# Payload rows as floats with both gates, multiplied and split per block on GpSimd, ScalarE and VectorE

## What is computed

```python
# x: (4, 3584, 192) -> attention -> (14336, 192)
logits = x @ phi                                 # 32 slots
d = softmax(logits, axis=0); c = softmax(logits, axis=1)
slot_out = experts(d.T @ x)                      # 8 experts, 4 slots each
x = c @ slot_out
noisy = x @ w_gate + log1p(exp(x @ w_noise)) * noise
top2, top2_w = two largest of noisy, softmax of the two
out[row] = sum over k of top2_w[row, k] * (relu(x[row] @ w1[e]) @ w2[e])
```

## Time and profile before

| | busy us | share of the span |
|---|---|---|
| TensorE matmul | 1046.8 | 91% |
| VectorE | 634.6 | 55% |
| ScalarE | 440.8 | 38% |
| GpSimd | 324.4 | 28% |

### The profile page before, as it was taken

One profiled execution on the slowest core, in us unless ns is written; L12 is line 12 of the kernel. 1 busy time (PEld: TensorE's weight loads), 2 busy tenths in 40 slices (PEclk: granted clock), 3 DMA queues, 4 the chain that ended last, 5 costly groups with the idle time before them and its releaser, 6 DMA issues.

```text
span 1149.5 us, 27573 instructions
## 1 busy us (share of the span) xinstructions
PE 1046.8 (91%) x8758; PEld 812.1 (71%) x8759; DVE 634.6 (55%) x1091; ACT 440.8 (38%) x818; POOL 324.4 (28%) x347
## 2 busy tenths in 40 slices
PE   6999899887886087999999999999999999999996
PEld 6999899713632035777777777777777777777774
DVE  3232542450379994656656655665666556655663
ACT  2222212110022453445544554454445444544453
POOL 4000000100001903443344334343433343334431
PEclk9999999989777588999999999999999999999999
DMA  6456765646242222333333333333333333333331
GB/s 203 154 177 205 248 198 200 192 132 194 59 110 62 120 99 59 112 109 109 109 106 112 109 106 106 108 113 104 109 111 103 113 106 112 110 106 106 111 113 39
DMA packets 76143, 142.29 MB, mean 124 GB/s; under 512 B 10876, under 2 KB 37804, under 8 KB 73800
## 3 DMA queue, kind: packets, MB, share of 16 engines
q1 hardware_dynamic: 64072, 120.72, 34.8%
q0 software_dynamic: 11120, 20.51, 6.1%
q10 hardware_dynamic: 912, 0.52, 0.2%
HBM read 67.70 MB, written 19.37 MB: 76 GB/s over the span
## 4 chain that ended last, share of the span: by engine, by line
PE 85%; DVE 6%; DMA 5%; issue 1%; ACT 1%; another core or an unknown queue 0%; POOL 0%; SPq 0%; PEldq 0%; ACTq 0%; POOLq 0%; DVEq 0%
PE ps L1156 32%; PE ps L1160 16%; PE ps L1145 11%; PE ps L950 8%; DMA stage<-in_moe_w 5%; PE ps L999 3%; PE ps L943 3%; PE ps L1001 2%; PE ps L1120 2%; PE ps L1031 2%; PE ps L1099 2%; PE ps L1135 1%; PE ps L1047 1%; PE ps L1082 1%; DVE gbuf L811 1%
## 5 line engine op out<-in xcount | busy, mean ns | idle before, releaser
L901 DVE SCALAR_TENSOR_TENSOR x_ring<-ps,x_ring 128x512 f16<-128x512 f32 x556 | 356.4, 682 | 275.4 <-ACT x_ring L557 163.6
L557 ACT ACTIVATE x_ring<-ps 128x512 f16<-128x512 f32 x556 | 302.4, 599 | 366.2 <-PE ps L1145 279.1
L1156 PE MATMUL ps<-w2hl,x_ring 128*128 x2224 | 408.7, 326 | 2.7 <-issue 1.4
L1156 PEld LDWEIGHTS ps<-w2hl,x_ring 128*128 128x128 f16 x2224 | 207.7, 97 | 113.8 <-issue 6.4
L444 POOL DMA_INDIRECT out_rows<-x_ring,row_id x139 | 137.2, 987 | 387.7 <-DVE x_ring L910 382.7
L1160 PE MATMUL ps<-w2hl,x_ring 128*128 x2224 | 228.9, 246 | 0.0
L1160 PEld LDWEIGHTS ps<-w2hl,x_ring 128*128 128x128 f16 x2224 | 191.3, 98 | 36.4 <-DVE x_ring L901 1.8
L1145 PE MATMUL ps<-c,x_ring 96*128 96x128 f16 x2224 | 170.9, 219 | 0.0
L438 POOL DMA_INDIRECT stage<-pay_rows,row_id x139 | 134.8, 970 | 77.5 <-DVE row_id L888 35.4
L1145 PEld LDWEIGHTS ps<-c,x_ring 96*128 96x128 f16 x2224 | 140.9, 98 | 0.0
L950 PE MATMUL ps<-phi_r,xT 96*128 96x224 f32 (+6 forms) x616 | 106.1, 321 | 0.0
(11 more groups left out here) (209 smaller groups left out, 651.1 us busy)
## 6 DMA issues: line engine op xcount, KB each, us to landing
x_ring<-a SPq DMA_DIRECT2D x278, 192.0 KB
stage<-in_moe_w SPq DMA_DIRECT2D x48, 768.0 KB, 7.9
x_ring<-in_x SPq DMA_DIRECT2D x14, 1536.0 KB, 6.6
pay_rows<-x_ring SPq DMA_DIRECT2D x4, 1344.0 KB, 4.6
stage<-pay_rows,row_id POOLq DMA_INDIRECT x139, 2.5
out_rows<-x_ring,row_id POOLq DMA_INDIRECT x139
gbuf<-in_moe_noise ACTq DMA_DIRECT2D x1, 448.0 KB, 5.7
x_halo<-in_x SPq DMA_DIRECT2D x4, 72.0 KB, 3.6
```

The source lines that it names most:

```text
L557: a.activation(hh[:, par, 4 * half:4 * half + 4, :].rearrange("p j q -> p (j q)"), ps[:, 2 + 2 * par + half, :], ACT.Relu).then_inc(hh_rea ...
L901: last = v.scalar_tensor_tensor(hl[:, par, 4 * half:4 * half + 4, :].rearrange("p j q -> p (j q)"), ps[:, 2 + 2 * par + half, :], 0.0, hh[ ...
L1156: t_.matmul(ps[:, 6 + b % 2, 0:2 * D], hh[:, k, j, :], w, start=k == 0 and j == 0, stop=False)
```

## The change

The payload row becomes 34 floats (136 bytes): the 32 numbers of c and the two gates. ScalarE copies lg into the tile cg (that takes the place of the payload quarters) and GpSimd writes the gates beside it from a reciprocal that VectorE leaves after the block tables; one DMA stores all. GpSimd also takes over the remainder of a3 from VectorE, reading a float copy a_f that ScalarE makes. The transposes of lg (quads) move between the steps of the earlier weights, into tiles of their own.

In the last loop GpSimd multiplies the gathered 32 numbers by both gates (gated, 128x64), ScalarE rounds and writes the result twice (split_high), VectorE subtracts (split_low); each stands LEAD = 3 blocks ahead of the block it serves. turn_c waits for split_low instead of the gather. In the changed kernel relu is L566, low_sum L572, split_high L579, low L893, row_sum L902, c_out L886, split_low L908, gather L441, multiplication L451, scatter L457.

```diff
         stage2 = sb("stage2", [P, T * NS])
         w2s = stage2[:, 0:2 * FJ * D].rearrange("p (a j d) -> p a j d", a=2, d=D)
-        ck = stage2[:, :].rearrange("p (a k t s) -> p a k t s", a=2, k=2, s=NS)
-        crow = stage2[:, 0:CR * KS].bitcast(F16).rearrange("p (a k) -> p a k", a=CR)
+        crow = stage2[:, 0:CR * KP].rearrange("p (a k) -> p a k", a=CR)
+        ck = stage2[:, CR * KP + 4 * KS:CR * KP + 4 * KS + 8 * NS].rearrange("p (a k s) -> p a k s", a=4, k=2)
+        csp = stage2[:, CR * KP:CR * KP + 4 * KS].bitcast(F16).rearrange("p (a k r s) -> p a k r s", a=4, k=2, s=NS)
         ident = sb("ident", [P, P])
...
-            sp.dma_start(pay[N:ROWS, :].rearrange("(p a) k -> p (a k)", a=4), zero16[:, :]).then_inc(zero_rows, 16)
-            for q in range(QT):
-                sp.wait_ge(pay_lo, 2 * q + 2)
-                sp.dma_start(pay[0:N, :].rearrange("(p t) k -> p t k", t=T)[:, q * TQ:(q + 1) * TQ, :],
-                             payload[:, q % 2, :, :]).then_inc(pay_out[q % 2], 16)
+            sp.dma_start(pay[N:ROWS, :].rearrange("(p a) k -> p (a k)", a=4),
+                         zero16[:, 0:2 * 4 * KP].bitcast(F32)).then_inc(zero_rows, 16)
+            sp.wait_ge(cg_ready, 1)
+            sp.wait_ge(gates_ready, 2)
+            sp.dma_start(pay[0:N, :].rearrange("(p t) k -> p t k", t=T), cg[:, :, :]).then_inc(pay_out, 16)
...
-            for a in range(2):
-                sp.wait_ge(pay_out[a], 8 * QT)
+            sp.wait_ge(pay_out, 16)
...
-            pool.wait_ge(gates_ready, 1)
-            def gated(q):
-                if q >= 2:
-                    pool.wait_ge(pay_lo, 2 * q - 2)
-                ts = slice(q * TQ, (q + 1) * TQ)
-                for k in range(2):
-                    g.tensor_tensor(ck[:, q % 2, k, :, :], lg[:, PAD + q * TQ:PAD + (q + 1) * TQ, :],
-                                    gm[:, 4 + k, ts].unsqueeze(2).to_broadcast([P, TQ, NS]), ALU.mult
-                                    ).then_inc(ck_ready, 1)
-            gated(0)
-            for q in range(QT):
-                if q + 1 < QT:
-                    gated(q + 1)
-                pool.wait_ge(ck_ready, 2 * q + 2)
-                for k in range(2):
-                    pool.wait_ge(pay_hi, 2 * q + k + 1)
-                    row = payload[:, q % 2, :, k * KS:(k + 1) * KS]
-                    g.tensor_tensor(row[:, :, 2 * NS:3 * NS], ck[:, q % 2, k, :, :], row[:, :, 0:NS], ALU.subtract
-                                    ).then_inc(pay_lo, 1)
+            for e in range(E):
+                if e:
+                    pool.wait_ge(a_lo, e)
+                pool.wait_ge(a_hi, e + 1)
+                pool.wait_ge(a_all, e + 1)
+                g.tensor_tensor(a3[NS:2 * NS, e, :], a_f[NS:2 * NS, :], a3[NS:2 * NS, e, :], ALU.subtract
+                                ).then_inc(a_lo, 1)
+            pool.wait_ge(a_lo, E)
+            pool.wait_ge(gate_inv, 1)
+            pool.wait_ge(sot_ps, 1)
+            step(g.tensor_scalar(gm[:, 0, :], gm[:, 3, :], C_SCALE, None, ALU.mult))
+            step(g.tensor_tensor(gm[:, 1, :], gm[:, 0, :], gm[:, 2, :], ALU.mult))
+            for k in range(2):
+                step(g.tensor_tensor(pr[:, 3, :], pr[:, 5 + k, :], gm[:, 0, :], ALU.mult))
+                step(g.tensor_tensor(pr[:, 4, :], pr[:, 6 - k, :], gm[:, 1, :], ALU.mult))
+                g.tensor_tensor(cg[:, :, NS + k], pr[:, 3, :], pr[:, 4, :], ALU.add).then_inc(gates_ready, 1)
+                pool.wait_ge(gates_ready, k + 1)
 
 
             def gather(n):
                 if n >= CR:
-                    pool.wait_ge(c3_ps, n - CR + 1)
+                    pool.wait_ge(ck_ready, n - CR + 1)
                 g.indirect_dma_start(crow[:, n % CR, :], None, pay[:, :],
                                      bass.IndirectOffsetOnAxis(ap=row_id[:, n:n + 1], axis=0)
                                      ).then_inc(g_in[n % CR], 16)
+
+            def gated(n):
+                pool.wait_ge(g_in[n % CR], 16 * (n // CR + 1))
+                if n:
+                    pool.wait_ge(ck_ready, n)
+                if n >= 4:
+                    pool.wait_ge(cs_lo, n - 3)
+                g.tensor_tensor(ck[:, n % 4, :, :], crow[:, n % CR, 0:NS].unsqueeze(1).to_broadcast([P, 2, NS]),
+                                crow[:, n % CR, NS:KP].unsqueeze(2).to_broadcast([P, 2, NS]), ALU.mult
+                                ).then_inc(ck_ready, 1)
...
-            for a in range(2):
-                pool.wait_ge(pay_out[a], 8 * QT)
+            pool.wait_ge(pay_out, 16)
             pool.wait_ge(tab_ready, 1)
             for n in range(CR - 2):
                 gather(n)
+            for n in range(LEAD):
+                gated(n)
             for n in range(NB):
                 if n + CR - 2 < NB:
                     gather(n + CR - 2)
+                if n + LEAD < NB:
+                    gated(n + LEAD)
                 scatter(n)
             for s in range(4):
                 pool.wait_ge(y_out[s], 16 * ((NB - 1 - s) // 4 + 1))
...
                 act.wait_ge(a_ps, e + 1)
                 a.activation(a3[:, e, :], ps[0:KS, 2 * (e % 2):2 * (e % 2) + 2, :].rearrange("p a f -> p (a f)"),
                              ACT.Copy).then_inc(a_hi, 1)
+                wait(act, a_lo, e)
+                a.activation(a_f[NS:2 * NS, :], ps[NS:2 * NS, 2 * (e % 2):2 * (e % 2) + 2, :].rearrange(
+                    "p a f -> p (a f)"), ACT.Copy).then_inc(a_all, 1)
+            act.wait_ge(sot_ps, 1)
+            a.activation(cg[:, :, 0:NS], lg[:, PAD:PAD + T, :], ACT.Copy).then_inc(cg_ready, 1)
...
-            def pay_high(q, k):
-                act.wait_ge(ck_ready, 2 * q + k + 1)
-                if q >= 2:
-                    act.wait_ge(pay_out[q % 2], 16 * (q // 2))
-                row = payload[:, q % 2, :, k * KS:(k + 1) * KS]
-                step(a.activation(row[:, :, 0:NS], ck[:, q % 2, k, :, :], ACT.Copy))
-                a.activation(row[:, :, NS:2 * NS], row[:, :, 0:NS], ACT.Copy).then_inc(pay_hi, 1)
...
-            for q in range(QT):
-                for k in range(2):
-                    pay_high(q, k)
...
+            def split_high(b, i):
+
+                act.wait_ge(ck_ready, i * BODY + (b + 1))
+                wait(act, c3_ps, i * BODY + (b - 3))
+                a.activation(csp[:, b % 4, :, 0:2, :], ck[:, b % 4, :, :].unsqueeze(2).to_broadcast([P, 2, 2, NS]),
+                             ACT.Copy).then_inc(cs_hi, 1)
+            for b in range(LEAD):
+                split_high(b, 0)
             relu(0, 0)
 
             def body(i, off, count, last):
                     relu(1, n * 2 + 1)
                     if b > 0:
                         low_sum((b - 1) % 2, n - 1)
+                    if not (last and b >= off + count - LEAD):
+                        split_high(b + LEAD, i)
                     if not (last and b == off + count - 1):
                         relu(0, n * 2 + 2)
...
+            for q in range(QGROUPS):
+                dve.wait_ge(ctT_ps, q + 1)
+                v.tensor_copy(cT(q), ps[:, 4 + q % 2, :]).then_inc(ctT_ready, 1)
...
+            a_scale()
             for q in range(QGROUPS):
-                if q == 2:
-                    a_scale()
-                dve.wait_ge(ctT_ps, q + 1)
-                if q >= 2:
-                    dve.wait_ge(gl_ps, q - 1)
-                v.tensor_copy(cT[:, q % 2, :], ps[:, 4 + q % 2, :]).then_inc(ctT_ready, 1)
-                if q:
-                    gl_out(q - 1)
-            gl_out(QGROUPS - 1)
-
-            def a_low(e):
-
-                dve.wait_ge(a_hi, e + 1)
-                v.tensor_tensor(a3[NS:2 * NS, e, :], ps[NS:2 * NS, 2 * (e % 2):2 * (e % 2) + 2, :].rearrange(
-                    "p a f -> p (a f)"), a3[NS:2 * NS, e, :], ALU.subtract).then_inc(a_lo, 1)
+                gl_out(q)
...
-            a_low(6)
-            dve.wait_ge(m_exp, 1)
-            step(v.tensor_scalar(gm[:, 3, :], gm[:, 2, :], 1.0, EPS, ALU.add, ALU.add))
-            step(v.reciprocal(gm[:, 3, :], gm[:, 3, :]))
-            step(v.tensor_scalar(gm[:, 0, :], gm[:, 3, :], C_SCALE, None, ALU.mult))
-            step(v.tensor_tensor(gm[:, 1, :], gm[:, 0, :], gm[:, 2, :], ALU.mult))
-            for k in range(2):
-                step(v.tensor_tensor(pr[:, 5, :], pr[:, k, :], pr[:, 1 - k, :], ALU.is_lt))
-                step(v.tensor_tensor(pr[:, 6, :], pr[:, 1 - k, :], pr[:, k, :], ALU.is_lt))
-                step(v.tensor_tensor(pr[:, 5, :], pr[:, 5, :], gm[:, 0, :], ALU.mult))
-                step(v.tensor_tensor(pr[:, 6, :], pr[:, 6, :], gm[:, 1, :], ALU.mult))
-                last = v.tensor_tensor(gm[:, 4 + k, :], pr[:, 5, :], pr[:, 6, :], ALU.add)
-                if k == 0:
-                    step(last)
-            last.then_inc(gates_ready, 1)
...
-            a_low(7)
             dve.wait_ge(eid_ps, 1)
             v.tensor_copy(eid[:, :].rearrange("p (b k) -> p k b", k=2),
```

(35 more changed lines are left out.)

45 lines of the change are left out of this document (17 added, 28 removed).

## The result

The changed kernel takes 1350.74 us, the median of 4 runs (1346.6 to 1355.59); the kernel before takes 1140.25 us beside it (1136.17 to 1149.48). The ratio is 1.1834, with a 95% interval of 1.175 to 1.1918. So it is slower by 210 us, where the prediction had 270.

What follows compares the result with a forecast made beforehand. TensorE, 91% busy, bounded the kernel before; the change adds a per-block round trip through GpSimd's queue. +285 us in the loop and -15 ahead made +270: 1411 us on the median, 1421 profiled, range 1310 to 1530.

Steps and rivals of the forecast that it cites:

- The cycle: Last loop: row_sum, scatter, gather, multiplication, split_high, relu and remainders wait in turn, 7.10 us a block instead of 4.99, +285 us.
- gather 0.97, and 0.30 until the next instruction, which is the same gap as between scatter and gather: Last loop, GpSimd: time from gather start to multiplication start, 1.27 us of the cycle.
- The main case: Last loop: a cycle of 6.7 to 7.7 us, time 1350 to 1500 us, predicted 1411; chance 0.66.
- the rival of a shorter cycle: Last loop: 6.2 to 6.6 us because hand-overs overlap or GpSimd's issue returns early, 1315 us and above; chance 0.10.
- Ahead of the loop: Everything before the last loop: -7.1 to the count, -15.8 to the one-hot work, gates +2.4, first block +5.2; sum -15.3 us.
- I charge each of six GpSimd remainders in full, 2.1 us: +12.6: Ahead of the count: VectorE loses the full length of six remainders handed to GpSimd, 12.6 us lost for 10.6 won.
- The rule of the Trainium skill quoted in the prediction: GpSimd and VectorE operations, fast two-port or with two SBUF inputs, exclude one another for a whole instruction.
- Gates: Beside the one-hot work: eight GpSimd operations on 128x112 at 0.3 us each, +2.4 us.
- The first block: Start of the last loop: six gather issues, then multiplication, rounding, remainder and transposes, 9.6 us instead of 4.4, +5.2.
- TensorE's clock: Last loop: idling 2 us of every 7 lowers the granted clock; a mixture near 8.3 us, 1572 us; chance 0.08.
- Dearer changes between computing and transfers on GpSimd: Last loop: switching costs extra, 1546 us at 1 us a block, 1479 at 0.5; chance 0.13 for over 7.8 us.
- The round trip hidden: Last loop: GpSimd's product arrives within the relu's 1.7 us of slack, so it costs nothing, 1126 us; chance 0.03.

Runs made afterwards that it cites:

- e1_mul_ahead: Changed kernel with GpSimd's multiplication four blocks ahead instead of three, ScalarE's and VectorE's splits still three ahead: 1125.49 us, 0.9852 of the kernel before.
- e4_before_tick: Kernel before, plus one GpSimd product of constants behind each gather, which ScalarE awaits before the next block's relu: 1359.36 us, ratio 1.1896.
- f1_rem_dve: e1_mul_ahead with the eight remainders of a3 back on VectorE and ScalarE's float copies dropped: 1123.3 us, 0.9855 of the kernel before.
- f2_quads_back: e1_mul_ahead with the transposes of lg back at their old place among the gate products: 1127.82 us, 0.9888 of the kernel before.
- e3_mul_first: Changed kernel with GpSimd's order in a body as product, gather, scatter instead of gather, product, scatter: 1178.59 us, 1.0327 of the kernel before.

## Why the prediction was right, and where its sizes were off

**Direction and cause: right, and shown.** Each sign that the prediction named is there: scatter, gather and product back to back on GpSimd, split_high waiting 3.79 us for them, relu(0) 0.22 us after it starts, TensorE idle 1.3 us a block (forecast 2) and at 81% (forecast some 75%, of a longer span), and the one-hot work earlier. e1_mul_ahead and e4_before_tick show that the wait is the cause.

**The cycle: 6.66 us, not 7.10.** Term by term, forecast and then measured in the block above:

| term | forecast | measured |
|---|---|---|
| row_sum to scatter | 0.69 | 0.69 |
| scatter to gather | 1.30 | 1.33 |
| gather to product | 1.27 | 0.99 |
| product, hand-over, until split_high | 0.42 | 0.34 |
| split_high to relu | 0.30 | 0.22 |
| relu to low(0) | 0.72 | 0.61 |
| low(0), low(1) to row_sum | 2.40 | 2.48 |

The step that failed is "gather 0.97, and 0.30 until the next instruction, which is the same gap as between scatter and gather". The gap belongs to two indirect transfers in a row; a product behind a gather starts 0.02 us after it. The nearest row of the trace was taken for a case of another kind, which is two thirds of the miss. The others are differences of at most 0.11 us, of both signs. In the usual turn of 6.60 us the last term is 2.42, so that the sum was 0.50 too long. The average over the loop is still a little lower (6.56 us), since the last six turns take 5.4 down to 2.5 us.

In the traces the loop grew by 218.1 us where the sum had 285, so 67 us less, and the part ahead of it shrank by 7.5 us more than forecast. Together that is the 75 us between the 1421 us given for the profiled execution and its 1346.6. For the median the miss is only 60 us (1411 against 1350.74), for a reason that has nothing to do with the sum (see below).

The main case, a cycle of 6.7 to 7.7 us, was given 0.66, and the cycle did not fall in it: 6.60 lies at the upper edge of the rival of a shorter cycle (6.2 to 6.6, given 0.10), whose mechanism, hand-overs that overlap, is close to what the trace shows. That the time still lies in the main case's 1350 to 1500 us, by 0.7 us, is luck.

**Ahead of the loop: -21.5 us, not -15.3** (from L1074 on; the other 1.3 of the 22.8 is where the last load stage ended). Its steps:
- VectorE goes on after the count at 356.00, forecast 361.9. The step that failed is "I charge each of six GpSimd remainders in full, 2.1 us: +12.6". By the lengthened operations it is about 7.8: L798 and L802 0.7 each, one L799 1.8, L806 1.1, the scan L817 1.8 and the copy L820 1.7 above what they take alone. The gain at this point is 11.6 us from L1074 on, where 7.1 was forecast. The time at which VectorE was to go on without any lock, 355.7, was also too late: the seventh product (now L1100) ended at 351.74, and TensorE then waited 3.17 us for the count. Why the charge was too high: part of the remainders ran beside reductions, which are not held up. The rule of the Trainium skill quoted in the prediction makes just this distinction, and the sum did not.
- From there to the one-hot work are 20.2 us (356.25 to 376.49) where 36.6 were, -16.3 against the forecast of -15.8, though two parts of it were off. L840 was to fall to 3.4 us, but lasts 5.37 with GpSimd's next work at 376.75, the same in f1_rem_dve, and 5.45 before: this pass is slow by itself, and wasn't held up before. It reads its tile across the classes and not in the order in which it is stored; whether that is the reason no run tests. And of the small operations L824 and L839 still lie beside the two late remainders (1.93 and 1.84 us). The other small ones take 0.15 to 0.28 us (0.44 for the cast of 278 elements), and pay for it.
- The one-hot work starts at 376.49, forecast near 383.
- Gates: eight GpSimd operations take 0.51 to 0.80 us, not 0.3, beside the one-hot work. The stretch from there to the first gather is 34.6 us where it was 33.3: +1.4, forecast +2.4.
- The first block: from the first gather (411.12) to L1146 (420.84) are 9.7 us; forecast 9.6.
- The remainders handed over gain nothing, as weighed: f1_rem_dve. The transposes' move is worth 2.5 to 3.9 us, forecast 4.5: f2_quads_back.

**The profiled execution and the median.** The profiled execution before took 1151.28 us, 11 more than the median of 1140.25 beside the changed kernel. The profiled changed kernel, by contrast, is the fastest of its four runs, 4 us under its median. So the traces differ by 195 us and the medians by 210. These 15 us work in favour of the forecast for the median; they say nothing about its terms.

**The rivals.** TensorE's clock: granted 1.00 from 560 to 700 us with 80% busy, so 1.3 us of idle time in each block (27.78 of the 140 us), and 0.99 over the whole loop. It falls as the cause of the loss, but the clock did move: it was 0.66 from 475 to 480 us and 0.67 from 495 to 500. In both cases it was at the lower of its two levels (a granted clock of 0.50, or 1.2 GHz) for about 3 us, behind idle gaps of TensorE of 1.8 and 1.4 us, and from 505 us on it was 1.00. The turn with the first fall took 6.66 us and the one behind the second 7.05, so the two cost less than a microsecond of the 210.

Dearer changes between computing and transfers on GpSimd: 0.02 us from a gather's end to the product's start, and in e3_mul_first 0.16 from the product's end to the gather's start; it falls. The round trip hidden: not in this kernel, but e1_mul_ahead is that case, made by the condition that the rival named (the product ahead of the scatter it stands behind), and takes 1125 us where 1126 was worked out.
